# Attention, a dense layer and an expert layer on one core: every engine's part of an attention unit is given a slot of its own, and two other orders are changed with it

## The chip, the core and the metric

The kernel runs on one core of a Trainium2 chip. The core has five engines, each with an instruction queue of its own that is worked off in order: TensorE (PE), VectorE (DVE), ScalarE (ACT), GpSimd (POOL) and SyncE (SP), the last of which only issues transfers here. The metric is the device time of one execution in microseconds (us), lower is better. Engines wait for one another by semaphores alone, and the kernel writes each of these waits out by hand.

## What is computed

The reference, cut to what matters: a linear attention over 8 batches of 8 heads, a dense layer with `h - tanh(h)` in the middle, and a layer of 8 experts in which each token goes to one expert.

```python
q_s = softmax(q, axis=-1);  k_s = softmax(k, axis=2)        # q, k, v: (8, 8, 576, 64)
kv  = einsum('bhsd,bhde->...', k_s^T v);  a = q_s @ kv      # per head
x   = a.transpose(0, 2, 1, 3).reshape(4608, 512)
h   = x @ w_in;  x = (h - tanh(h)) @ w_out                  # 512 -> 2048 -> 512
logits = normed(x) @ normed(expert_emb).T / tau
e = argmax(logits);  gate = softmax(logits)[e]
out[n] = gate[n] * (relu(x[n] @ w1[e[n]]) @ w2[e[n]])       # 512 -> 1024 -> 512
```

All tensors are float32. Each matrix product of the two layers is done as three products of a high part and a low part (`split3`, lines 528 to 532: high times high, high times low, low times high), which keeps the accuracy of float32.

## The kernel before, in words

**Two halves.** The first half joins attention, dense layer and routing in one stream; the second is the expert layer.

**Slots.** The dense layer is cut into 12 blocks of 384 tokens and each block into 16 chunks of 128 of the 2048 inner columns: 192 chunks, one for each slot. In slot `s` PE does the first product of chunk `s+2` (12 matmuls of 384 columns), the second product of chunk `s` (9 matmuls of 512 columns), then what attention and routing have for it. ACT and DVE do the elementwise work of chunk `s+2`: on ACT a square, a tanh, a second square, the rounding of the chunk before to `g_hi`, and a mask (lines 799 to 811); on DVE four operations (lines 1000 to 1008). POOL makes `g_lo` of chunk `s+1` (L1397). The second product waits for `g_lo`; the first product of a chunk waits for the last DVE operation of the chunk two before. A turn of 48 slots (`SUPER`) covers three blocks, that is two batches. `walk` (line 370) writes out 16 slots, then a loop of three turns, then the last 32 slots.

**Attention units.** A unit is two heads of one batch; there are 32. Units 0 to 4, and the first steps of unit 5, are done in a prologue, whose order is the list `PROLOGUE`; the others lie beside the dense layer. `unit_at` (line 283) gives each of them four slots in a row: the eight units of a turn take slots 28 to 47 and 0 to 11, and slots 12 to 27 have none. Within the four slots `STAGES` (line 83) says what is done in which, the same for PE, DVE and POOL, with a shorter list for ACT. A `+` means the next unit:

- slot 0: `qa` (PE turns half of q, ACT copies it), `kT` (PE turns the folded k, DVE takes the maximum, L1032), `qmax` of the next unit (DVE maximum L1019, POOL subtracts it L1408)
- slot 1: `row` (PE spreads the maximum, DVE subtracts it L1035, ACT exponential L828), `qb` (the other half of q), `qexp` of the next unit (ACT L831)
- slot 2: `kv` (PE 12 pairs of small matmuls L602, DVE scales them L1039 to L1045), `qsum` of the next unit (DVE L1022 to L1026, POOL multiplies L1412)
- slot 3: `out` (PE two matmuls L608 and L609, ACT rounds both halves L834 and L836, DVE takes the rests L1049 and L1052), `kfold` of the next unit (DVE L1029)

All units share two accumulator banks, A and Bk. In the last turn the steps with `+` run once more, for a unit 32 that does not exist, on data that SP loads a second time for it.

**Routing.** The block that has just been finished is routed in the 16 slots of the next one. `ROUTE` gives each step its slot: three times `turn`, `pieces`, `logits`, with PE, ACT and DVE handing one bank to and fro (L620, L849, L1069, L852, L1072, L640), then `choose` on DVE in slot 9, `ranks` in slot 10, `dest` on DVE in slot 11 (L1107 to L1118), and one scatter of 128 rows on POOL in each of the slots 11, 12 and 13 (L1424). In slot 15 POOL waits until the scatters have landed and says so with `rows_free`; ACT waits for that before it writes the next block's rows into the same tile (`rows_out`, line 857).

**The order inside a slot** is the same on each engine: elementwise work, then attention, then routing. In the first 12 slots of all, ACT and DVE also split ten pieces of the weights (`SPLITS`, L869 and L1132).

**The expert layer** has 37 tiles of 128 rows that are live. PE does for tile `t`: first half of the hidden product of `t+1`, the transposes of `t` (L713), those of `t+2` (L685), second half of the hidden product of `t+1`, second product of `t`. DVE does for tile `t`: a test whether weights are to be split, `h_split` (L1219), `t_split` of `t+2` (L1213), more tests and splits of weights (L1337), then `scaled` (L1346), which waits for the second product and writes the output tile. In a loop of seven rounds four tiles are written out; the jump back to its top stands on DVE between `scaled` of one tile and `h_split` of the next.

Of the kernel before, what the change touches and what calls it, by code (L numbers as in the profile page):

```python
# [80 lines left out]
    "w:4 emb:0 first:0 kv:4 qmax:5 w:5 qa:4 first:1 qb:4 qexp:5 emb:1 qsum:5 out:4 kfold:5").split())]  # L81

STAGES = ("qa", "kT", "qmax+"), ("row", "qb", "qexp+"), ("kv", "qsum+"), ("out", "kfold+")
STAGES_ACT = (("qa",), ("qb", "row", "qexp+"), (), ("out",))
# [11 lines left out]
         11: ("dest", "scatter:0"), 12: ("scatter:1",), 13: ("scatter:2",), 15: ("stored",)}  # L96
# [23 lines left out]
def build(nc, q, k, v, w_in, w_out, emb, tau, w1, w2, ident_d, tri_d, cst_d, rows_d, pad_d, out):  # L120
# [91 lines left out]
    def unit_bufs(u, par):  # L212
# [42 lines left out]
    rows_free, route_step, oneh_ready, shift_ready, p_exp, rank_ready, dest_ready, rows_stored = (  # L255
        sem(x) for x in ("rows_free", "route_step", "oneh_ready", "shift_ready", "p_exp", "rank_ready", "dest_ready", "rows_stored"))
# [26 lines left out]
    def unit_at(m, s):  # L283

        if s >= 28:
            j = 2 * UPB + (s - 28) // 4
        elif s < 12:
            j = UPB + 1 + s // 4
        else:
            return None  # L290
        if isinstance(m, int) and 2 * UPB * m + j >= UNITS:
            return None
        return m * (2 * UPB) + j, s % 4, j // UPB % 2, j % UPB, j % 2
# [56 lines left out]
    def steps_of(stages, u, stage_, hf, c, par, part):  # L350

        for x in stages[stage_]:
            if x[-1] == "+":
                part(x[:-1], u + 1, hf, c, 1 - par)
            else:
                part(x, u, hf, c, par)

    def prologue(part, piece_, first, emb_):

        for x, i in PROLOGUE:  # L360
            if x == "w":
                piece_(i)
            elif x == "first":
                first(i)
            elif x == "emb":
                emb_(i)
            else:
                part(x, i, i // UPB, i % UPB, i % 2)
# [25 lines left out]
    def _(sp):  # L394
# [71 lines left out]
        sp.wait_ge(q_normed, UNITS + 1)  # L466
        sp.wait_ge(kfolded, UNITS + 1)
# [57 lines left out]
    def _(pe):  # L525
# [38 lines left out]
        def attention(m, s):  # L564
            at_ = unit_at(m, s)
            if at_:
                attention_stage(*at_)

        def attention_stage(u, stage_, hf, c, par):
            steps_of(STAGES, u, stage_, hf, c, par, part)  # L570

        def part(what, u, hf, c, par):

            q_, k_, v_, kv_, qT_, kfold_, _, _, kmax_, _, bankA, bankB = unit_bufs(u, par)
            if what == "qa":
                pe.wait_ge(q_normed, u + 1)
                if not isinstance(u, int) or u >= UPB:
                    pe.wait_ge(xlo_b, u + 1)
# [3 lines left out]
            elif what == "kT":  # L582
                pe.wait_ge(kfolded, u + 1)
                if not isinstance(u, int) or u >= UPB:
                    pe.wait_ge(xlo_a, u)
                nc.tensor.transpose(bankA[:, 0:SP], kfold_[:], ident[0:SP, 0:SP]).then_inc(kmaxT_ready, 1)
            elif what == "row":

                pe.wait_ge(kmax_done, u + 1)
                nc.tensor.transpose(bankA[0:SP, 0:P], kmax_[:, 0:1].broadcast_to([P, SP]),  # L590
# [76 lines left out]
        def slot(m, s):  # L667
# [3 lines left out]
            attention(m, s)  # L671
# [106 lines left out]
    def _(act):  # L778
# [34 lines left out]
        def attention_stage(u, stage_, hf, c, par):  # L813
            steps_of(STAGES_ACT, u, stage_, hf, c, par, part)

        def part(what, u, hf, c, par):
# [15 lines left out]
            elif what == "out":  # L832
                act.wait_ge(oa_ready, u + 1)
                nc.scalar.copy(x_hi[:, c, col:col + HALF], bankA[:, 0:HALF]).then_inc(xhi_a, 1)  # L834
                act.wait_ge(ob_ready, u + 1)
# [21 lines left out]
        def rows_out(m, s):  # L857
# [3 lines left out]
            act.wait_ge(rows_free, j + 1)  # L861
# [11 lines left out]
        def slot(m, s):  # L873
# [4 lines left out]
            at_ = unit_at(m, s)  # L878
            if at_:
                attention_stage(*at_)  # L880
# [101 lines left out]
    def _(dve):  # L982
# [27 lines left out]
        def attention_stage(u, stage_, hf, c, par):  # L1010
            steps_of(STAGES, u, stage_, hf, c, par, part)

        def part(what, u, hf, c, par):
# [16 lines left out]
            elif what == "kT":  # L1030
                dve.wait_ge(kmaxT_ready, u + 1)
                V.tensor_reduce(kmax_[:, 0:1], bankA[:, 0:SP], axis=AX.X, op=ALU.max).then_inc(kmax_done, 1)  # L1032
# [14 lines left out]
            elif what == "out":  # L1047
                dve.wait_ge(xhi_a, u + 1)
                V.tensor_tensor(x_lo[:, c, col:col + HALF], bankA[:, 0:HALF],  # L1049
                                x_hi[:, c, col:col + HALF].bitcast(F32), ALU.subtract).then_inc(xlo_a, 1)  # L1050
                dve.wait_ge(xhi_b, u + 1)
# [114 lines left out]
        def slot(m, s):  # L1166
# [4 lines left out]
            at_ = unit_at(m, s)  # L1171
            if at_:
                attention_stage(*at_)
# [175 lines left out]
        def slot(t, j, ahead1, ahead2, stored):  # L1349
            with live(dve, t):  # L1350
                if ahead1:

                    weights(t, T_SOLE, range(4))
                h_split(t, j)
                if ahead2:
                    with live(dve, t + 2):
                        t_split(t + 2, (j + 2) % 4)
# [136 lines left out]
```

## Time and profile before

| | us |
|---|---|
| median of 3 runs (1533.52 to 1538.3) | 1535.5 |
| the profiled execution | 1540.79 |
| its span, first to last instruction | 1539.0 |
| PE busy in the span | 1442.9 (94%) |
| DVE busy | 920.7 (60%) |
| ACT busy | 768.3 (50%) |
| POOL busy | 397.7 (26%) |
| mean granted clock of PE, as a share of full speed | 0.981 |

The slot work runs from 61 us to about 1025 us of the span, the expert layer from there to the end. A busy time is the sum of the durations of an engine's instructions where they do not overlap. Matmuls overlap, since one starts before the one ahead has ended, so short waits of PE don't show in its busy time; they show in the distance between starts.

### The profile page before, as it was taken

What the parts mean: (1) busy time and instruction counts of PE and PEld (TensorE: products, weight loads), DVE (VectorE), ACT (ScalarE), POOL (GpSimd) and SP (SyncE); (2) the same over time, 40 slices, a digit from 0 to 9 for tenths busy, and PEclk for the clock granted to TensorE, in tenths of its full rate; (3) what the DMA queues carried; (4) which work ended last, traced back from release to release, by engine and by line L of the source; (5) the groups of instructions that cost most, each with busy time, mean ns of one, the idle gap of its engine ahead of it and who ended that gap; (6) DMA issues with size and microseconds to landing.
All of it is one profiled execution on the core that took longest, in us unless ns stands there. A gap on an engine that the chain in (4) does not pass through costs nothing.

```text
span 1539.0 us, 27343 instructions
## 1 busy us (share of the span) xinstructions
PE 1442.9 (94%) x8080; PEld 1226.6 (80%) x8081; DVE 920.7 (60%) x1784; ACT 768.3 (50%) x1559; POOL 397.7 (26%) x348
## 2 busy tenths in 40 slices
PE   4799999999999999999999999999999899899996
PEld 3678888888888888888888888877888778678785
DVE  7886677878577878667887766675314123232221
ACT  3666666675657666656666566652323123132220
POOL 3433233334233343324333323231000000000000
PEclk9899999999999999999999999998999999999999
DMA  9532012212001221101121002025312211311110
GB/s 193 148 94 79 1 45 47 64 36 53 9 25 44 47 68 34 37 1 52 42 65 40 22 1 76 1 97 193 116 44 90 94 42 53 131 34 47 41 39 25
DMA packets 139524, 91.18 MB, mean 59 GB/s; under 512 B 118873, under 2 KB 119129, under 8 KB 139233
## 3 DMA queue, kind: packets, MB, share of 16 engines
q1 hardware_dynamic: 132784, 70.12, 17.1%
q0 software_dynamic: 5840, 18.92, 3.3%
q8 instruction: 64, 1.05, 0.3%
q14 instruction: 100, 0.81, 0.2%
q10 hardware_dynamic: 736, 0.29, 0.1%
HBM read 70.39 MB, written 21.28 MB: 60 GB/s over the span
## 4 chain that ended last, share of the span: by engine, by line
PE 56%; DVE 22%; issue 10%; ACT 6%; POOL 3%; DMA 1%; DVEq 1%; ACTq 1%; SPq 0%; POOLq 0%
PE ps L530 17%; PE ps L531 17%; PE ps L532 17%; DVE gs L1003 5%; DVE gs L1000 2%; DVE kfold L1029 2%; ACT gs L804 2%; DVE gs L1008 2%; PE ps L713 2%; DVE k_sb L1035 2%; DVE qrec L1022 1%; POOL g_lo L1397 1%; DVE ps L1001 1%; ACT q_sb L831 1%; PE ps L685 1%
## 5 line engine op out<-in xcount | busy, mean ns | idle before, releaser
L1397 POOL TENSOR_TENSOR g_lo<-gs,g_hi 128x384 fp32r<-128x384 f32 x192 | 205.3, 1069 | 420.2 <-ACT g_hi L809 419.0
L530 PE MATMUL ps<-x_hi,wi_hi 128*128 128x384 f32 x768 | 277.0, 361 | 0.8 <-issue 0.8
L531 PE MATMUL ps<-x_lo,wi_hi 128*128 128x384 f32 x768 | 261.4, 340 | 0.0
L532 PE MATMUL ps<-x_hi,wi_lo 128*128 128x384 f32 x768 | 261.2, 340 | 0.0
L530 PE MATMUL ps<-wo_hi,g_hi 128*128 128x512 f32 x576 | 233.1, 405 | 26.5 <-POOL g_lo L1397 26.2
L531 PE MATMUL ps<-wo_lo,g_hi 128*128 128x512 f32 x576 | 231.0, 401 | 0.0
L532 PE MATMUL ps<-wo_hi,g_lo 128*128 128x512 f32 x576 | 229.6, 399 | 0.0
L799 ACT ACTIVATE usq<-ps 128x384 f32<-128x384 f32 x192 | 93.8, 488 | 250.8 <-PE ps L532 250.8
L920 ACT ACTIVATE hb<-ps 128x512 f32<-128x512 f32 x74 | 44.3, 598 | 330.9 <-PE ps L532 330.9
L1000 DVE SCALAR_TENSOR_TENSOR gs<-gs,ps 128x384 f32<-128x384 f32 x192 | 106.0, 552 | 169.0 <-ACT gs L804 167.5
L1003 DVE TENSOR_TENSOR gs<-gs,usq 128x384 f32<-128x384 f32 x192 | 175.4, 914 | 0.0
L530 PEld LDWEIGHTS ps<-wo_hi,g_hi 128*128 128x128 f32 x576 | 109.5, 190 | 54.9 <-POOL g_lo L1397 24.1
L1466 POOL DMA_INDIRECT out<-osb,xrow x37 | 36.2, 979 | 448.1 <-DVE osb L1346 431.0
L530 PEld LDWEIGHTS ps<-x_hi,wi_hi 128*128 128x128 f32 x768 | 145.8, 190 | 5.9 <-issue 1.7
L531 PEld LDWEIGHTS ps<-x_lo,wi_hi 128*128 128x128 f32 x768 | 145.9, 190 | 2.9
L532 PEld LDWEIGHTS ps<-x_hi,wi_lo 128*128 128x128 f32 x768 | 145.4, 189 | 0.0
L1346 DVE TENSOR_SCALAR osb<-ps,xrow 128x512 f32<-128x512 f32 x37 | 27.8, 750 | 188.5 <-PE ps L532 188.5
L530 PE MATMUL ps<-w_hi,h_hi 128*128 (+1 forms) x296 | 120.6, 408 | 18.3 <-DVE h_lo L1219 18.3
L1008 DVE COPY_PREDICATED gs<-big,ps 128x384 f32<-128x384 uint16 x192 | 114.3, 595 | 34.0 <-DVE gs L1003 34.0
L532 PEld LDWEIGHTS ps<-wo_hi,g_lo 128*128 128x128 f32 x576 | 109.6, 190 | 26.8
L530 PE MATMUL ps<-w_hi,t_hi 128*128 (+1 forms) x296 | 122.0, 412 | 2.6 <-issue 2.6
L531 PEld LDWEIGHTS ps<-wo_lo,g_hi 128*128 128x128 f32 x576 | 109.3, 190 | 17.5
(209 smaller groups left out, 2698.8 us busy)
## 6 DMA issues: line engine op xcount, KB each, us to landing
w_raw<-w SPq DMA_DIRECT2D x10, 2048.0 KB, 9.0
xrow<-scratch SPq DMA_DIRECT2D x37, 257.0 KB, 2.7
q_sb<-q SPq DMA_DIRECT2D x62, 144.0 KB, 3.0
k_sb<-k SPq DMA_DIRECT2D x62, 144.0 KB, 3.1
v_sb<-v SPq DMA_DIRECT2D x60, 144.0 KB, 3.3
in_raw<-w_in SPq DMA_DIRECT2D x8, 512.0 KB, 5.9
out_raw<-w_out SPq DMA_DIRECT2D x8, 512.0 KB, 5.6
scratch<-pad_d SPq DMA_DIRECT2D x8, 257.0 KB, 4.5
```

Source lines behind the costliest of these rows:

```text
L530: mm(out_, a_hi, b_hi, start=first, stop=False)
L531: mm(out_, a_hi, b_lo, start=False, stop=False)
L532: return mm(out_, a_lo, b_hi, start=False, stop=last)
L713: last = nc.tensor.transpose(ps[:, 3 + b, i * P:(i + 1) * P], hb[:, j % 2, (4 * b + i) * P:(4 * b + i + 1) * P], ident[:])
L799: fn(usq[:, s % 2], h, ACT.Square).then_inc(u_ready, 1)
L804: fn(gs[:, s % 2], usq[:, s % 2], ACT.Square, bias=cst[:, C_BIAS:C_BIAS + 1], scale=SQ_SCALE).then_inc(s_ready, 1)
L920: fn(hb[:, j % 2, 512 * hf:512 * (hf + 1)], ps[:, 1 + hf], ACT.Relu).then_inc(relu_done, 1)
L1000: V.scalar_tensor_tensor(g, g, SQ_REST, h, ALU.add, ALU.mult).then_inc(poly_step, 1)
L1003: V.tensor_tensor(g, g, u, ALU.mult).then_inc(poly_ready, 1)
L1008: V.copy_predicated(g, big[:].bitcast(U16), h).then_inc(g_ready, 1)
L1397: G.tensor_tensor(g_lo[:, (s - 1) % 3], gs[:, (s - 1) % 2], g_hi[:, (s - 1) % 3].bitcast(F32), ALU.subtract).then_inc(glo_ready, 1)
L1466: G.indirect_dma_start(out, bass.IndirectOffsetOnAxis(ap=xrow[:, j, DEST:DEST + 1].bitcast(U32), axis=0), osb[:, j], None, bounds_check=N ...
```

## The change

Attention no longer goes by stages of four slots. A table `EVENTS` names for each engine its operations and, for each, a distance in slots from the unit's last slot, called `t`. A unit now spreads over eight slots, from `t-6` to `t+1`. `out` is cut in two: `outa` at `t`, `outb` at `t+1`. The operations of one engine follow in the order of its row; an operation of POOL or ACT lies one slot or more behind that of DVE or PE whose result it takes, and the other way round, in most cases.

| operation | slots before, from `t` | slots after |
|---|---|---|
| `qmax` | -7 | DVE -6, POOL -5 |
| `kfold` | -4 | DVE -5 |
| `qexp` | -6 | ACT -4 |
| `kT` | -3 | PE, DVE -4 |
| `qsum` | -5 | DVE -4, POOL -3 |
| `row` | -2 | PE, DVE -3, ACT -2 |
| `qa` | -3 | PE, ACT -2 |
| `qb` | -2 | PE, ACT -1 |
| `kv` | -1 | PE, DVE -1 |
| `out` | 0 | first half 0, second half +1 |

`kT` now uses bank Bk, and the waits on the banks follow from that: `row` waits until `outa` of the unit before is read, `outb` until the maximum of the unit behind it is taken. The prologue ends with `kT:5`. The steps for unit 32 and their loads are gone, and SP loads the first expert's weights when the last unit has been read. In routing `dest` moves from slot 11 to 12, the scatters from 11, 12, 13 to 13, 13, 14; POOL's wait in slot 15 is gone, and ACT waits for the scatters itself. In the expert layer DVE's loop begins elsewhere: its body is `scaled` of a tile and then the splits of the next, so that the jump back stands between the splits of a tile and its `scaled`. The order of DVE's work is the same.

The diff, cut to its core:

```diff
-    "w:4 emb:0 first:0 kv:4 qmax:5 w:5 qa:4 first:1 qb:4 qexp:5 emb:1 qsum:5 out:4 kfold:5").split())]
-STAGES = ("qa", "kT", "qmax+"), ("row", "qb", "qexp+"), ("kv", "qsum+"), ("out", "kfold+")
-STAGES_ACT = (("qa",), ("qb", "row", "qexp+"), (), ("out",))
+    "w:4 emb:0 first:0 kv:4 qmax:5 w:5 qa:4 first:1 qb:4 qexp:5 emb:1 qsum:5 out:4 kfold:5 kT:5").split())]
+EVENTS = dict(
+    PE=(("kT", -4), ("row", -3), ("qa", -2), ("qb", -1), ("kv", -1), ("outa", 0), ("outb", 1)),
+    ACT=(("qexp", -4), ("row", -2), ("qa", -2), ("qb", -1), ("outa", 0), ("outb", 1)),
+    DVE=(("kT", -4), ("qsum", -4), ("row", -3), ("qmax", -6), ("kv", -1), ("kfold", -5), ("outa", 0), ("outb", 1)),
+    POOL=(("qmax", -5), ("qsum", -3)))
...
-         11: ("dest", "scatter:0"), 12: ("scatter:1",), 13: ("scatter:2",), 15: ("stored",)}
+         12: ("dest",), 13: ("scatter:0", "scatter:1"), 14: ("scatter:2",)}
...
-    def unit_at(m, s):
+    def attention(engine, m, s, part):
+        for what, after in EVENTS[engine]:
+            turn, t = divmod(s - after, SUPER)
+            if t % 4 != 3 or 12 <= t < 28:
+                continue
+            j = 2 * UPB + (t - 28) // 4 if t >= 28 else UPB + 1 + t // 4
+            if isinstance(m, int) and not UPB < (m + turn) * 2 * UPB + j < UNITS:
+                continue
+            part(what, (m + turn) * (2 * UPB) + j, j // UPB % 2, j % UPB, j % 2, t)
...
-        sp.wait_ge(qTb_ready, UNITS - 1)
-        load(q_sb[:, 0], q_d, q_in, 0, 0)
-        sp.wait_ge(kv_ready, UNITS - 1)
-        load(k_sb[:, 0], k_d, k_in, 0, 0)
...
-        sp.wait_ge(q_normed, UNITS + 1)
-        sp.wait_ge(kfolded, UNITS + 1)
+        sp.wait_ge(qTb_ready, UNITS)
+        sp.wait_ge(kv_ready, UNITS)
         sp.wait_ge(first_known, 1)
...
             if what == "qa":
                 pe.wait_ge(q_normed, u + 1)
+                pe.wait_ge(kmax_done, u + 1)
...
             elif what == "kT":
                 pe.wait_ge(kfolded, u + 1)
+                if t in (None, 31):
+                    if u >= UPB if isinstance(u, int) else True:
+                        pe.wait_ge(xlo_b, u + 1)
+                else:
+                    pe.wait_ge(qTb_copied, u)
+                nc.tensor.transpose(bankB[:, 0:SP], kfold_[:], ident[0:SP, 0:SP]).then_inc(kmaxT_ready, 1)
+            elif what == "row":
+                pe.wait_ge(kmax_done, u + 1)
                 if not isinstance(u, int) or u >= UPB:
                     pe.wait_ge(xlo_a, u)
-                nc.tensor.transpose(bankA[:, 0:SP], kfold_[:], ident[0:SP, 0:SP]).then_inc(kmaxT_ready, 1)
...
-            elif what == "out":
+            if what in ("outa", "out"):
                 pe.wait_ge(kvb_ready, u + 1)
+                pe.wait_ge(qTa_copied, u + 1)
+                mm(bankA[:, 0:HALF], kv_, qT_[:, 0:HALF], start=True, stop=True).then_inc(oa_ready, 1)
+            if what in ("outb", "out"):
                 pe.wait_ge(qTb_copied, u + 1)
-                mm(bankA[:, 0:HALF], kv_, qT_[:, 0:HALF], start=True, stop=True).then_inc(oa_ready, 1)
+                if t not in (None, 11):
+                    pe.wait_ge(kmax_done, u + 2)
                 mm(bankB[:, 0:HALF], kv_, qT_[:, HALF:S], start=True, stop=True).then_inc(ob_ready, 1)
...
-            act.wait_ge(rows_free, j + 1)
+            if not isinstance(j, int) or j > 0:
+                act.wait_ge(rows_stored, j * (16 * GPB))
...
-        slot(3, 3, True, True, None)
+        splits(3, 3, True, True)
+        scaled(3, 3, None)
+        splits(4, 0, True, True)
         with dve.Fori(1, LOOPS) as i:
             for j in range(4):
-                slot(i * 4 + j, j, True, True, i * 16)
+                scaled(i * 4 + j, j, i * 16)
+                splits(i * 4 + (j + 1), (j + 1) % 4, True, True)
+        scaled(4 * LOOPS, 0, 16 * LOOPS)
```

`splits` is the old DVE `slot` of the expert layer without its last line, the call of `scaled`. ACT, DVE and POOL split their `part` for `out` in the same way as PE.

## Rows read from the trace of the kernel before

**Rows 1.** Waits of PE over the whole span: us in total, times, longest.

```profile
PE ps L530 <- POOL g_lo L1397: 26.2, 26, 2.4
PE ps L530 <- DVE h_lo L1219: 18.3, 7, 5.8
```

**Rows 2.** Stretches: from:to, length, busy us of PE, PEld, DVE, ACT, POOL, clock, DMA.

```profile
61.24:137.69 76.45, 68.20 (x383) 57.57 (x383) 63.17 (x106) 47.16 (x92) 33.37 (x20) 0.96 0.34 91
203.88:396.91 193.03, 184.36 (x1160) 159.06 (x1160) 151.57 (x314) 122.11 (x263) 73.36 (x63) 0.99 0.20 50
296.06:315.80 19.74, 19.74 (x121) 17.44 (x121) 15.13 (x30) 14.50 (x32) 9.38 (x8) 1.00 0.28 75
450.42:641.80 191.38, 182.64 (x1160) 157.97 (x1160) 151.54 (x314) 122.00 (x263) 73.16 (x63) 1.00 0.20 51
695.20:887.52 192.32, 183.97 (x1160) 159.19 (x1159) 151.63 (x314) 122.04 (x263) 73.19 (x63) 0.99 0.17 44
887.52:958.25 70.73, 70.67 (x394) 62.89 (x394) 46.67 (x102) 43.36 (x96) 20.52 (x20) 1.00 0.11 38
949.82:958.25 8.43, 8.43 (x43) 7.61 (x43) 5.70 (x15) 6.04 (x13) 2.02 (x2) 1.00 0.72 251
```

**Rows 3.** Timeline of DVE, a third slot of a unit and the fourth behind it.

```profile
263.27 0.14 DVE L1039 TENSOR_SCALAR krec<-ps 128x1 f32<-128x1 f32 x1
...
264.26 0.95 DVE L1022 TENSOR_REDUCE qrec<-q_sb 96x12 f32<-96x768 f32 x1
...
265.81 0.55 DVE L1000 SCALAR_TENSOR_TENSOR gs<-gs,ps 128x384 f32<-128x384 f32 x1
...
268.30 0.44 DVE L1049 TENSOR_TENSOR x_lo<-ps,x_hi 128x288 fp32r<-128x288 f32 x1
...
269.02 1.54 DVE L1029 TENSOR_REDUCE kfold<-k_sb 96x128 f32<-96x768 f32 x1
```

**Rows 4.** Timeline of DVE, first operation on a chunk in the slot from 949.82.

```profile
951.42 0.55 DVE L1000 SCALAR_TENSOR_TENSOR gs<-gs,ps 128x384 f32<-128x384 f32 x1 [0.73 <-ACT gs L804]
```

**Rows 5.** Timeline of ACT, DVE and PE, first hand-overs of a block's routing.

```profile
235.29 0.84 ACT L828 ACTIVATE k_sb<-k_sb 96x768 f32<-96x768 f32 x1 [2.23 <-DVE k_sb L1035]
...
237.37 0.70 DVE L1069 TENSOR_TENSOR ps<-ps,y 128x512 f32<-128x512 f32 x1 [2.11 <-ACT y L849]
...
244.37 0.29 PE L640 MATMUL ps<-en,y 128*128 128x24 bf16 x5 [0.84 <-DVE y L1072]
```

**Rows 6.** Timeline of POOL and PE, scatter of a block and the slot behind it.

```profile
379.70 1.06 POOL L1424 DMA_INDIRECT scratch<-yrow,dest  x1 [4.39 <-DVE dest L1118]
...
381.85 0.74 PE L530 MATMUL ps<-wo_hi,g_hi 128*128 128x512 f32 x1 [2.01 <-POOL g_lo L1397]
```

**Rows 7.** Timeline of PE and DVE, end of the prologue and first slot.

```profile
57.11 0.94 PE L530 MATMUL ps<-x_hi,wi_hi 128*128 128x384 f32 x1
...
62.22 1.55 DVE L1029 TENSOR_REDUCE kfold<-k_sb 96x128 f32<-96x768 f32 x1
63.70 1.21 DVE L1132 TENSOR_TENSOR wi_lo<-in_raw,wi_hi 128x1024 fp32r<-128x1024 f32 x1
```

**Rows 8.** The line of the 36 scatters (L1424), its transfers.

```profile
DMA to landing us min/median/max: 3.3/3.9/8.0
```

**Rows 9.** Stretches of the expert layer: 22 tiles with the jumps, 3 without.

```profile
1141.09:1439.54 298.45, 282.90 (x1321) 230.55 (x1320) 84.47 (x100) 80.63 (x122) 21.54 (x22) 0.97 0.21 67
1452.04:1489.55 37.51, 37.51 (x182) 30.85 (x180) 7.92 (x12) 7.96 (x15) 2.94 (x3) 1.00 0.13 41
```

**Rows 10.** Chain that ended last, at a jump: start, us, what (DVEq: DVE's sequencer).

```profile
1198.19 3.12 issue
...
1202.12 5.44 issue
```

**Rows 11.** Timeline of DVE, a tile without a jump ahead of it.

```profile
1096.38 0.75 DVE L1346 TENSOR_SCALAR osb<-ps,xrow 128x512 f32<-128x512 f32 x1 [6.71 <-PE ps L532]
1100.28 1.29 DVE L1219 TENSOR_TENSOR h_lo<-ps,h_hi 128x512 fp32r<-128x512 f32 x2 [3.15 <-ACT h_hi L925]
```

More of the change, by code:

```diff
@@ L367, in prologue @@
             else:
-                part(x, i, i // UPB, i % UPB, i % 2)
+                part(x, i, i // UPB, i % UPB, i % 2, None)
     def walk(eng, slot, extra={}):
@@ L562, in second_product, with part @@
             last.then_inc(l2_done, 1)
[L564 to L572, printed above, removed]
+        def part(what, u, hf, c, par, t):
             q_, k_, v_, kv_, qT_, kfold_, _, _, kmax_, _, bankA, bankB = unit_bufs(u, par)
@@ L670, in slot @@
             second_product(m, s)
-            attention(m, s)
+            attention("PE", m, s, part)
             if isinstance(m, int) and m == 0 and s == AHEAD - 1:
@@ L831, in part @@
                 fn(q_, q_, ACT.Exp).then_inc(q_exp, 1)
-            elif what == "out":
+            if what in ("outa", "out"):
                 act.wait_ge(oa_ready, u + 1)
                 nc.scalar.copy(x_hi[:, c, col:col + HALF], bankA[:, 0:HALF]).then_inc(xhi_a, 1)
+            if what in ("outb", "out"):
                 act.wait_ge(ob_ready, u + 1)
@@ L877, in slot @@
             elementwise(m + (s + 2) // SUPER, (s + 2) % SUPER)
-            at_ = unit_at(m, s)
-            if at_:
-                attention_stage(*at_)
+            attention("ACT", m, s, part)
             at_ = route_at(m, s)
@@ L1046, in part @@
                 last.then_inc(kvb_ready, 1)
-            elif what == "out":
+            if what in ("outa", "out"):
                 dve.wait_ge(xhi_a, u + 1)
@@ L1050, in part @@
                                 x_hi[:, c, col:col + HALF].bitcast(F32), ALU.subtract).then_inc(xlo_a, 1)
+            if what in ("outb", "out"):
                 dve.wait_ge(xhi_b, u + 1)
@@ L1170, in slot @@
             elementwise(m + (s + 2) // SUPER, (s + 2) % SUPER)
-            at_ = unit_at(m, s)
-            if at_:
-                attention_stage(*at_)
+            attention("DVE", m, s, part)
             at_ = route_at(m, s)
@@ L1347, in scaled, with splits @@
                             ALU.mult).then_inc(o_ready, 1)
[L1349 to L1357, printed above, removed]
-                if ahead1:
-                    weights(t, T_NEW, (0, 1))
-                    weights(t, T_SECOND, (2, 3))
-                scaled(t, j, stored)
+        def splits(t, j, ahead1, ahead2):
+            if ahead1:
+                weights(t, T_SOLE, range(4))
+            h_split(t, j)
+            if ahead2:
+                with live(dve, t + 2):
+                    t_split(t + 2, (j + 2) % 4)
+            if ahead1:
+                weights(t, T_NEW, (0, 1))
+                weights(t, T_SECOND, (2, 3))
         dve.wait_ge(tab_ready, 1)
@@ L1375, in _ @@
         scaled(2, 2, None)
-        slot(3, 3, True, True, None)
+        splits(3, 3, True, True)
+        scaled(3, 3, None)
+        splits(4, 0, True, True)
         with dve.Fori(1, LOOPS) as i:
             for j in range(4):
-                slot(i * 4 + j, j, True, True, i * 16)
-        for t in range(4 * LOOPS, TILES):
-            slot(t, t % 4, t + 1 < TILES, t + 2 < TILES, 16 * (t // 4))
+                scaled(i * 4 + j, j, i * 16)
+                splits(i * 4 + (j + 1), (j + 1) % 4, True, True)
+        scaled(4 * LOOPS, 0, 16 * LOOPS)
+        for t in range(4 * LOOPS + 1, TILES):
+            with live(dve, t):
+                splits(t, t % 4, t + 1 < TILES, t + 2 < TILES)
+                scaled(t, t % 4, 16 * (t // 4))
     @block.gpsimd
@@ L1409, in part @@
                                 ALU.subtract).then_inc(q_centred, 1)
-            elif what == "qsum":
+            elif what == "qsum" and not (isinstance(u, int) and u == UPB + 1 and t is not None):
                 pool.wait_ge(qrec_ready, u + 1)
@@ L1443, in slot @@
             lo(mm_, s2)
-            at_ = unit_at(m, s)
-            if at_:
-                attention_stage(*at_)
+            attention("POOL", m, s, part)
             at_ = route_at(m, s)
```

39 lines of the change are left out of this document (6 added, 33 removed).

## The prediction, made before the changed kernel was run

> **What bounds the kernel now.** I read the stretches first, then PE's waits, then the timeline at the places where these end. PE is the bound: where a stretch has neither attention nor routing, two slots take 8.43 us, 4.22 each, and PE is busy for all of it [rows 2]. So time can be won only where PE stands still, and I measure that by lengths. Sixteen slots with routing and no attention take 70.73, so routing adds 70.73 - 16 x 4.22 = 3.2. Four slots of attention without routing and without a wait take 19.74, so a unit adds 19.74 - 4 x 4.22 = 2.86 [rows 2]. The three spans of 36 slots around the attention of a turn hold 8 units and 2 routings each: 36 x 4.22 + 8 x 2.86 + 2 x 3.2 = 181.2. They take 193.0, 191.4 and 192.3 [rows 2], which leaves 11.8 + 10.2 + 11.1 = **33.1 us** of standing still. The first 13 slots hold 3 units and no routing: 54.9 + 8.6 = 63.5 against 76.45, so **13.0**. In the expert layer three tiles take 37.51, 12.50 each; the 22 tiles from 1141.09 on take 298.45 where 22 x 12.50 = 275.0 [rows 9]: **23.4**. PE's waits have two large entries, for POOL's `g_lo` and for DVE's `h_lo` [rows 1]; the first belongs to the slots, the second to the expert layer.
>
> DVE comes close behind. It is busy for 151.6 of 193.0 us in a span, 79% [rows 2]. As starts go, an elementwise chunk takes 268.30 - 265.81 = 2.49 of it, `kv` 0.99, `qsum` 1.55 with 0.1 of that a routing step, `out` 0.72 [rows 3], `kfold` 63.70 - 62.22 = 1.48 [rows 7]; `row` and `qmax` are one pass over 96 x 768 elements like L1022, 0.9 each.
>
> **Where the spans stand still.** First hand-over: ACT waits 2.23 for DVE's `row` of the same slot, then does both exponentials, 0.84 each, and only then routing's copy, so DVE waits 2.11 for that copy, and PE 0.84 for `logits` seven microseconds on [rows 5]. Second: `dest` ends late because `out`, `kfold` and `dest` meet in slot 11 on DVE; POOL waits 4.39 with its scatter at the head of the queue, `g_lo` stands behind it, and PE waits 2.01 for that [rows 6].
>
> **The change, spans.** Per four slots DVE's attention work was, in order, 1.1, 0.9, 2.4, 2.2. Now it is 1.3 (`row`, `outb`), 0.9 (`qmax`), 2.5 (`kv`, `kfold`), 2.0 (`kT`, `qsum`, `outa`): the same sum, as even as before. What is better is what it meets. `dest` (some ten small operations, 0.14 and a gap each like L1039 [rows 3], so 1.5 to 2, an estimate) falls on a slot with 1.3 instead of 2.2, and the scatters one slot later find it done, so POOL no longer stands with `g_lo` behind it. ACT's exponential of k finds its input a slot old, the other exponential is in another slot, and routing's copy no longer queues behind a wait. POOL's `qsum` no longer waits in the slot in which DVE makes it. I then went through each wait of PE with a slot of 4.9 to 5.5 and DVE's first operation 1.6 after PE's slot begins (951.42 against 949.82 [rows 2, 4]): `kT`, `qa`, `qb`, `kv`, `outa` and `outb` each find their inputs 1 us old or more. The closest is `row`, which needs `outa` of the unit before out of the bank: DVE is through with it 1.6 + 2.5 + 2.0 = 6.1 after the slot begins, PE comes for it at 4.9 + 2.1 = 7.0. DVE's worst slot is the one with `choose` (2.5 + 0.9 + some 2.3 for ten linked small operations, 5.7 against 4.9 for PE), and the next ones give that back. So I keep 1.5 of stall per span and take 33.1 - 4.5 = **28.6 us**. Bounds: 33.1, and half, 16.
>
> **The change, start.** Here it costs something first. The prologue now ends with `kT:5`, and on PE this stands ahead of the first product of chunk 2, which started at 57.11; it needs `kfold:5`, which DVE runs from 62.22 to 63.8 [rows 7]. PE stands for 6.8 us, and resumes at 1.2 instead of 2.4 GHz, as it had it here anyway: from 57.11 to the next product at 61.24 its 12 matmuls took 4.1 us, where 4.22 is otherwise enough for 21 [rows 2, 7]. The second product of chunk 0 moves from 61.24 to about 68. But DVE uses these microseconds for two pieces of the weights that were in the way later, and POOL's two waits no longer stand before `g_lo`. Taking slot by slot the later of PE (4.22 and its attention) and of DVE (2.5, attention, 1.2 for each weight piece [rows 7]), I get 82.6 for the start of slot 3, 103.4 for slot 7, 128.3 for slot 12 and 133.1 for slot 13, which was at 137.69: **4.6 us** won of 13.0. Bounds: -4 (the delay is kept) and 9.
>
> **Scatters and the end of the slots.** Each scatter takes 3.9 us to land, up to 8.0 [rows 8]. The third one is now issued in slot 14, after POOL's `qmax` where there is one, and ACT waits for its landing itself in slot 15 before `rows_out`; behind ACT's wait stands the next chunk's square, and behind the copies PE's second product of the next slot. With 3.9 it lands about 1 us after ACT asks, with PE still 1 us short of needing the copies: no cost inside the turns. At the last block nothing follows that could absorb it, the weights of the first expert load at the same time, and the scatter behaves like the 8.0 one: I charge **-2 us** (bounds 0 and -5). The removed work for unit 32 lay beside a full PE and saves nothing; SP's first weight load still waits for `first_known`, which was the later condition.
>
> **Expert layer.** At six places DVE jumps back between `scaled` and `h_split`. In an ordinary tile `h_split` starts 3.90 after `scaled` and the 3.15 before it are spent waiting for ACT [rows 11]. At a jump two gaps of issue come in between, 3.12 and 5.44 at the longest [rows 10], and PE waits, 18.3 in seven waits [rows 1], the seventh being the last tile, which stays. Moved behind the splits, the jump falls into the 6.71 us that DVE waits for the second product anyway [rows 11]; the output tile has a tile's time to spare. All of 23.4 goes, and I take **22.5**, with 16 as the lower bound: the second gap stands at the test for weights (the jump over a skipped block), and that test still follows `scaled`.
>
> That second gap is where a page speaks against the change. The Trainium skill, "Runtime: NRT & Kernel Launch", section Instruction fetch mechanics, says that prefetch is sequential and that a taken branch to a target outside the current window of two pages forces a fetch before execution goes on. By it the skip over the weight block costs its fetch wherever it stands, and only the first gap is hidden. The trace agrees that both jumps have a gap; whether the second needs the first ahead of it, it does not show.
>
> Sum: 28.6 + 4.6 - 2 + 22.5 = 53.7. The profiled execution took 1540.8, so 1487.1; the median lies 5.3 below that execution, so **1482**.
>
> **Rivals.** (a) *DVE holds the spans.* Its in-order waits come back at other places, `choose` and the pairs of `kv` and `kfold` push its elementwise work late, and half of the 33.1 stays. For it: 79% busy, and its share rises to 84% when the span shrinks. Against: only the slot with `choose` holds clearly more work for DVE than for PE. 28.6 becomes 16: 1494. (b) *The second gap stays in the expert layer.* At the jump of rows 10 the second gap ends at 1207.56; 3.12 earlier is 1204.4, 6.2 behind the begin of the first gap, where an ordinary `h_split` stands 3.9 behind `scaled`, so it is still 2.4 late [rows 10, 11]; a gap of 3.12 or less fits into the 3.15. Over the six jumps I keep a quarter of 23.4, 6 us: 1488. The Trainium skill's page named above, "Runtime: NRT & Kernel Launch", gives this case. (c) *The shared bank.* `row` of a unit waits on PE until DVE has read `outa` of the one before, which it does last of three operations. Slack is 0.9. If DVE runs 2.9 us late there, PE stands 2.0 per unit, and a product at half clock behind it costs some 2 more (the 4.1 above against half of it): 27 units x 4 = 108 us, 1482 + 108 = 1590. It passes the old time from a loss of 53.5 / 27 = 2.0 us per unit on. Against: DVE's lateness adds up to 0.8 in my count. (d) *Nothing to speak of*: what the spans win is lost at the start and at the end, and the fetch keeps its place: 1535.
>
> **How the numbers follow.** My forecast 0.60, (a) 0.18, (b) 0.13, (c) 0.05, (d) 0.04. The low end takes all upper bounds, 33.1 + 9 + 23.4 = 65.5, so 1470, and 2 for the spread of runs: 1468. The high end is (a) and (b) together, 1500, with 3 for the last block: 1503. A measurement of this kernel tells 0.3% from no change, about 5 us. Faster: forecast, (a), (b) and a little of (d), 0.92; same 0.03; slower 0.05.
>
> **What would show it.** PE's waits without L1219 except once; the 22 tiles 275 to 277 long. Three spans of 36 slots (now with their events from slot 25 on) 182 to 184 long, no wait for `g_lo` behind a scatter. One wait of 6 to 7 us at `kT` (L586 before) near 57 us, and slot 13 at about 133. ACT waiting for the scatter at the last block. Wrong would be: waits of PE at `row`, a DVE without gaps through the spans, issue gaps still ahead of `h_lo`.

## The result, and the profile after

The changed kernel takes **1485.7 us** (median of four runs, 1484.5 to 1490.0) against 1534.5 for the one before in the same session (four runs, 1533.0 to 1538.3): ratio 0.9683, with a 95% interval of 0.9656 to 0.9710. The forecast was 1482, with a range of 1468 to 1503. The profiled execution took 1489.95 us, 50.8 less than the one of before (1540.8), and the terms below are differences between these two.

I read the same stretches as before, each set between two events that both kernels have. The three spans of attention are taken from slot 25 to slot 64 of their turn here, since the new events begin earlier than the old stages. First, stretches of the kernel before, the three spans and the last 15 slots ahead of the last one (from:to, length, busy us of PE, PEld, DVE, ACT, POOL, clock, DMA):

```profile
190.48:396.91 206.43, 197.76 (x1244) 170.85 (x1244) 161.28 (x338) 129.09 (x279) 76.38 (x66) 0.99 0.19 47
437.02:641.75 204.73, 195.99 (x1244) 169.71 (x1244) 161.26 (x338) 128.98 (x279) 76.20 (x66) 1.00 0.19 47
681.86:887.52 205.66, 197.31 (x1243) 170.93 (x1243) 161.29 (x338) 129.03 (x279) 76.22 (x66) 0.99 0.16 41
958.25:1023.45 65.20, 63.27 (x353) 54.99 (x352) 42.72 (x86) 39.88 (x86) 21.04 (x19) 1.00 0.11 31
```

Then stretches of the changed kernel: the first 13 slots, the three spans, the 16 slots with routing alone, the 15 slots behind them, the 22 expert tiles:

```profile
66.50:130.09 63.59, 63.59 (x381) 56.40 (x381) 53.47 (x93) 45.21 (x90) 20.85 (x17) 0.99 0.38 106
182.88:378.69 195.81, 193.43 (x1244) 170.86 (x1243) 163.30 (x338) 126.99 (x279) 78.61 (x66) 1.00 0.20 50
418.78:614.05 195.27, 193.49 (x1243) 170.84 (x1243) 162.03 (x338) 126.68 (x279) 78.32 (x66) 1.00 0.20 50
654.16:849.96 195.80, 193.49 (x1244) 170.91 (x1243) 162.09 (x338) 126.55 (x279) 78.39 (x66) 1.00 0.16 40
849.96:924.35 74.39, 70.57 (x395) 62.82 (x394) 47.09 (x102) 42.60 (x95) 20.62 (x20) 1.00 0.12 40
924.35:992.22 67.87, 64.42 (x353) 56.37 (x353) 44.20 (x87) 42.82 (x89) 20.26 (x18) 0.97 0.09 25
1110.37:1385.41 275.04, 275.04 (x1322) 226.36 (x1320) 84.21 (x100) 80.65 (x122) 21.52 (x22) 1.00 0.22 72
```

The spans lost 10.6, 9.5 and 9.9 us, 29.9 together; PE now stands still in them for 2.4, 1.8 and 2.3 (length less busy), where it was 8.7, 8.7 and 8.4; the rest of the gain is in PE's busy time itself, 193.5 for 197.0 on average, since a short wait doesn't show as one. The expert tiles take 275.04 for 298.45 [rows 9], and PE is busy for every microsecond of them: 23.4 won. Slot 13 begins at 130.09 instead of 137.69 [rows 2]: 7.6 won. One stretch went the other way: the 16 slots with routing alone take 74.39 instead of 70.73 [rows 2]; the 15 slots behind them take 67.87 where it was 65.2, so the end of the slots costs 6.3 in all. From the second product of the last expert tile to the end of the span it is 18.5 us instead of 15.3, 3.1 more. Added up: 7.6 + 29.9 - 6.3 + 23.4 - 3.1 = 51.5, within 0.7 of the 50.8.

Two of these terms compare one execution with one, and other runs vary there. The prologue before slot 0 is the same in `before` as in three runs shown below (before_pad, rot_only, route_only), and slot 0 begins at 61.24 in the one and at 58.80, 58.95 and 58.99 in the others. PE's lines of before and before_pad:

```profile
61.24 0.40 PE L530 MATMUL ps<-wo_hi,g_hi 128*128 128x512 f32 x1
58.80 0.40 PE L530 MATMUL ps<-wo_hi,g_hi 128*128 128x512 f32 x1
```

So some 2.3 of the 7.6 us belong to the profiled execution of before and not to the change, which leaves about 5.3 for the change. And the stretch from the last second product to the end is 15.0 to 15.3 us in eight of the profiled runs and 17.0 to 18.5 in the six others. Of the ten with the new events four are in the first group (no_rot 15.2) and six in the second (events_only 18.1); the four with the old ones are all in the first, so whether the change has a part in it stays open. PE waits 2.7 us for `h_lo` ahead of it before and after the change; the six microseconds from its begin have a granted clock of 0.72 after and of 1.00 before:

```profile
1469.44:1475.44 6.00, 6.00 (x19) 4.78 (x20) 0.00 (x0) 0.00 (x0) 0.00 (x0) 0.72 0.08 29
1523.69:1529.69 6.00, 5.86 (x24) 4.42 (x24) 0.11 (x1) 0.00 (x0) 0.00 (x0) 1.00 0.07 24
```

Waits of PE in the changed kernel (us in total, times, longest), which answer to [rows 1]:

```profile
PE ps L571 <- DVE kfold L1014: 25.3, 9, 9.0
PE ps L519 <- ACT yrow L853: 5.4, 4, 3.8
PE ps L640 <- DVE oneh L1089: 4.2, 4, 1.5
PE ps L519 <- POOL g_lo L1384: 3.5, 2, 2.6
PE ps L519 <- DVE h_lo L1203: 2.7, 1, 2.7
```

POOL's `g_lo` fell from 26 waits to two, both in the last block, and `h_lo` from seven to the one of the last tile. New is a wait for `yrow`, ACT's copies of the next block's rows: 3.8 us at the end of the slots, and 1.6 us in three short waits inside the turns. The first entry is the prologue, and in it the wait at `kT:5` that was forecast as 6.8 us. Timeline of PE at that place:

```profile
62.38 0.42 PE L571 MATMUL ps<-ident,kfold 96*128 96x96 f32 x1 [6.97 <-DVE kfold L1014]
```

Where the end of the slots loses time, the timeline of ACT and PE (slot 176 of 191), then of POOL, DVE and ACT in the last block:

```profile
923.62 1.56 ACT L853 COPY yrow<-ps 128x512 f32<-128x512 f32 x3 [4.99 <-DMA scratch<-yrow,dest]
924.35 0.72 PE L519 MATMUL ps<-wo_hi,g_hi 128*128 128x512 f32 x1 [3.82 <-ACT yrow L853]
...
988.00 2.29 DVE L1165 TENSOR_TENSOR w_lo<-w_raw,w_hi 128x2048 fp32r<-128x2048 f32 x1
988.37 2.76 POOL L1408 DMA_INDIRECT scratch<-yrow,dest  x1 [0.30 <-issue]
992.04 2.29 DVE L1165 TENSOR_TENSOR w_lo<-w_raw,w_hi 128x2048 fp32r<-128x2048 f32 x1 [1.11 <-ACT w_hi L878]
992.22 0.50 PE L519 MATMUL ps<-wo_hi,g_hi 128*128 128x512 f32 x1 [2.62 <-POOL g_lo L1384]
992.33 2.87 POOL L1408 DMA_INDIRECT scratch<-yrow,dest  x1 [0.17 <-issue]
999.32 1.56 ACT L853 COPY yrow<-ps 128x512 f32<-128x512 f32 x3 [7.30 <-DMA scratch<-yrow,dest]
```

And the timeline of SP and POOL 9 us ahead of the first of these waits:

```profile
914.19 0.41 SPq L450 DMA_DIRECT2D w_raw<-w  x1
915.14 1.12 POOL L1408 DMA_INDIRECT scratch<-yrow,dest  x1 [0.16 <-issue]
```

The third scatter of the block is issued 0.95 us after the first 2 MB load of expert weights and is through at 923.6, some 8.5 us later, where the median was 3.9 [rows 8]. ACT waits 4.99 for it, PE 3.82 for ACT, and PE then works at a granted clock of 0.72 for the next 5 us, so partly at 1.2 instead of 2.4 GHz:

```profile
925.00:930.00 5.00, 5.00 (x20) 4.29 (x19) 2.47 (x4) 4.42 (x12) 1.01 (x1) 0.72 0.01 3
```

In the last block two scatters take POOL 2.8 us each, beside DVE's split of weights, where the usual one took 1.06 [rows 6]; each ends some 0.85 us behind DVE's operation.

### The profile page after: what moved, and what is told of

Same layout as the page of the kernel before. It is cut to its first block, busy times and chain, and to the rows that moved or that the text cites. A ratio compares the mean times of both kernels' runs of the same rounds, so it can differ in the third digit from the quotient of the medians.

```text
span 1487.9 us, 27350 instructions
## 1 busy us (share of the span) xinstructions
PE 1421.7 (96%) x8080; PEld 1223.4 (82%) x8081; DVE 920.1 (62%) x1779; ACT 759.4 (51%) x1558; POOL 395.3 (27%) x346
## 3 DMA queue, kind: packets, MB, share of 16 engines
q1 hardware_dynamic: 130416, 69.53, 17.9%
## 4 chain that ended last, share of the span: by engine, by line
PE 79%; DVE 7%; issue 6%; POOL 3%; DMA 3%; ACT 1%; SPq 0%; DVEq 0%; POOLq 0%; ACTq 0%
PE ps L519 24%; PE ps L520 23%; PE ps L521 23%; PE ps L704 2%; DMA scratch<-yrow,dest 2%; PE ps L589 1%; POOL g_lo L1384 1%; PE ps L676 1%; PE ps L611 1%; PE ps L600 1%; DVE gs L991 1%; PE ps L595 1%; DMA xrow<-scratch 1%; DVE kfold L1014 1%; POOL q_sb L1392 1%
## 5 line engine op out<-in xcount | busy, mean ns | idle before, releaser
L1384 POOL TENSOR_TENSOR g_lo<-gs,g_hi 128x384 fp32r<-128x384 f32 x192 | 194.6, 1014 | 590.4 <-ACT g_hi L800 590.3
L519 PE MATMUL ps<-x_hi,wi_hi 128*128 128x384 f32 x768 | 280.1, 365 | 1.1 <-issue 1.1
L519 PE MATMUL ps<-wo_hi,g_hi 128*128 128x512 f32 x576 | 229.7, 399 | 8.9 <-ACT yrow L853 5.4
```

Source lines behind the costliest of these rows:

```text
L519: mm(out_, a_hi, b_hi, start=first, stop=False)
L1384: G.tensor_tensor(g_lo[:, (s - 1) % 3], gs[:, (s - 1) % 2], g_hi[:, (s - 1) % 3].bitcast(F32), ALU.subtract).then_inc(glo_ready, 1)
```

## The experiments

The experiments ran in three sessions, in which the kernel before gave medians of 1535.1, 1536.3 and 1534.3 us; each ratio is against the one it ran with. Differences of some 5 us between two experiments are near what the intervals of the ratios can tell; where one is used below, the trace is asked too.

### The parts one by one

**rot_only**: the kernel before with the new beginning of DVE's expert loop.

```diff
-                slot(i * 4 + j, j, True, True, i * 16)
+                scaled(i * 4 + j, j, i * 16)
+                splits(i * 4 + (j + 1), (j + 1) % 4, True, True)
```

> The kernel before with DVE's expert loop begun elsewhere and nothing else. Theory (the jump's gaps are hidden behind the wait for the second product): the 22 tiles from the second product of tile 7 to that of tile 29 take 275 to 276 us instead of 298.5, the slots are untouched, the time falls by 22 to 24 us to about 1512. Rival (b) (the gap at the test for weights stays behind scaled): 281 us or more for the 22 tiles, time 1518 or more, and issue gaps ahead of h_lo.

1514.3 us, ratio 0.9865 (0.9830 to 0.9899). The tiles all take 12.50, the slots are as before. That fits a jump whose gaps are hidden; it fits gaps that are gone just as well, and the next part shows that they were gone.

**route_only**: the kernel before with `dest` and the scatters later and ACT waiting for them itself.

```diff
-         11: ("dest", "scatter:0"), 12: ("scatter:1",), 13: ("scatter:2",), 15: ("stored",)}
+         12: ("dest",), 13: ("scatter:0", "scatter:1"), 14: ("scatter:2",)}
...
-            act.wait_ge(rows_free, j + 1)
+            if not isinstance(j, int) or j > 0:
+                act.wait_ge(rows_stored, j * (16 * GPB))
```

> The kernel before with dest and the scatters one slot later and ACT waiting for the scatters itself; attention in its old stages, expert loop as before. Theory (two causes in the spans: dest and the scatter at the head of POOL's queue, and hand-overs inside a slot): the waits for g_lo in slots 44, 60 and 61 of a turn go, some 4 to 5 us for each turn, the waits at logits stay (6.4 us in the span); at the last two blocks 5 to 7 us are lost to late scatters. Time 1534.5 - 13 + 6 = 1527, between 1522 and 1533. Rival: the events alone bring the gain and this part is worth nothing: 1538 or more.

1568.1 us, ratio 1.0214 (1.0187 to 1.0241): slower by 33 us, and not faster by 8. The timeline of POOL, ACT and PE, two slots of the first turn, shows why:

```profile
221.15 1.47 POOL L1412 TENSOR_TENSOR q_sb<-q_sb,qrec 96x768 f32<-96x768 f32 x1 [3.57 <-DVE qrec L1027]
222.78 1.14 POOL L1424 DMA_INDIRECT scratch<-yrow,dest  x1 [0.16 <-issue]
226.27 1.56 ACT L864 COPY yrow<-ps 128x512 f32<-128x512 f32 x3 [4.86 <-DMA scratch<-yrow,dest]
226.91 0.50 PE L530 MATMUL ps<-wo_hi,g_hi 128*128 128x512 f32 x1 [3.81 <-ACT yrow L864]
```

With the old stages POOL's `qsum` waits 3.57 for DVE in the very slot in which the third scatter now is, and the scatter goes out behind it, at 222.78. The new slots of the scatters are right only with the new events, in which POOL's `qsum` has its input already.

**route_old**: the changed kernel with `dest` and the scatters in their old slots 11, 12 and 13.

```diff
-         12: ("dest",), 13: ("scatter:0", "scatter:1"), 14: ("scatter:2",)}
+         11: ("dest", "scatter:0"), 12: ("scatter:1",), 13: ("scatter:2",)}
```

> The changed kernel with dest in slot 11 and the scatters in 11, 12, 13 again, ACT still waiting for them itself. Theory: in the spans POOL waits for dest again with g_lo behind it, but dest now meets 2.0 of attention work on DVE instead of 2.2, so 3 to 5 us are lost per turn, 9 to 14 in all; at the last two blocks 6 us are won back. Time 1485.7 + 12 - 6 = 1491, between 1486 and 1497. Rival (the later slots only cost, since the events have made room on DVE): 1482 or less.

1484.0 us, ratio 0.9657 (0.9628 to 0.9686), no slower than the changed kernel, and below the 1491 that was expected. The two halves cancel: in each turn two slots at a scatter take 5.8 and 5.7 where they took 4.3 and 4.8, at the end the 16 slots are back at 70.7.

**end_early** keeps the new slots in the turns and takes the old ones for the last two blocks.

```diff
-        for x in ROUTE.get(stage_, ()):
+        for x in (ROUTE_END if isinstance(j, int) and j >= NBLK - 3 else ROUTE).get(stage_, ()):
```

`ROUTE_END` is `ROUTE` with the old slots of these steps.

> The changed kernel, but dest and the scatters of the last two blocks of four units at their old slots (dest and first scatter in slot 11, then 12 and 13); all blocks in the turns keep the new slots. Theory LATE END (the second half of the change costs nothing in the turns and about 6 us behind them, where the scatters land behind the 2 MB load of w1 or beside DVE's weights): the wait of 3.8 us in slot 175 and those of the last block shrink, 1479 to 1481. Rival (the waits only move to another engine): 1484 to 1487.

1478.3 us, ratio 0.9622 (0.9593 to 0.9651): 7.5 below the changed kernel. Its stretches of the last 31 slots, ACT's waits for the scatters, and the same waits in the changed kernel:

```profile
848.00:918.70 70.70, 70.64 (x394) 62.90 (x394) 46.65 (x102) 43.32 (x96) 20.51 (x20) 1.00 0.11 39
918.70:983.90 65.20, 63.28 (x353) 55.04 (x352) 43.51 (x87) 40.71 (x87) 21.05 (x19) 1.00 0.11 30
```

```profile
ACT yrow L854 <- DMA scratch<-yrow,dest: 7.6, 9, 3.4
```

```profile
ACT yrow L853 <- DMA scratch<-yrow,dest: 18.9, 10, 7.3
```

So the later scatters gain 1484.0 - 1478.3 = 5.7 us in the turns and lose 7.5 behind them. The traces agree on the size: slots 0 to 159 take 789.8 us in route_old, 783.5 in the changed kernel and 781.6 in end_early, and the 31 slots behind them 135.9 in route_old and end_early against 142.3 in the changed kernel.

**events_only**: the changed kernel with both other parts undone, so the attention events alone (the edits of route_old, and the reverse of that of rot_only).

> The changed kernel with only the attention events new: DVE's expert loop and the slots of dest and the scatters are as before the change. The loop starts at 1632 of DVE's stream. If the events alone bring the three spans, the start and (by place) the expert layer: 1481 to 1485, tiles all 12.5 us, q14 near 68 packets. If the parts need one another (the earlier single undoings each covered for the other): 1490 to 1510.

1485.5 us, ratio 0.9682 (0.9666 to 0.9698), the whole gain of the change.

### The expert loop: where the wait went

**no_rot**: the changed kernel with DVE's expert loop as it was before.

> The changed kernel with DVE's expert loop as before. Theory: the parts are independent, the 22 tiles take 298 us again, the time is 1485.7 + 23.5 = 1509, within 3. If it were less than 1503 or more than 1515, the loop's gain would hang on what the slots do.

1484.6 us, ratio 0.9673 (0.9646 to 0.9700), not 1509. The tiles took 12.50 each although the jump stood in its old place. So the gaps had gone without any hiding, and the forecast's "hidden behind the 6.71 us" was not needed to explain the changed kernel.

The packets of queue q14, over which instructions are loaded, divided the kernels: 100 before and 98 in route_only, both with gaps, 68 or 69 in all without. I counted DVE's compiled instructions up to the top of the loop, which has 312 (313 when rotated): 1643 before and in route_only, 1632 in no_rot, 1695 after, 1706 in rot_only. The new events give DVE 11 instructions less, the rotation puts the top 63 later. So the runs are divided by the loop's place as well: gaps at 1643, none at 1632, 1695 and 1706.

The Trainium skill, "Runtime: NRT & Kernel Launch", section Instruction fetch mechanics, says that the instruction memory holds two blocks of 256 instructions and that a jump out of them forces a fetch. By it a loop of 312 that lies over three blocks can never stay in and one over two can. With the 256 of the Trainium skill's page the counts then bound the border B between two blocks, as an estimate: the loop from 1632 ends at 1943 and must end ahead of B + 256, so B is above 1687, and the loop at 1695 must not begin ahead of it, so B is at most 1695. Three kernels tested the place: the kernel before, no_rot and the changed kernel, each with a block ahead of the loop whose condition is false, so that only the loop's place is moved, to 1704, 1653 and 1912:

```diff
+        with dve.If(entry(0, T_SECOND, 1) > 0):
+            for _ in range(55):
+                hold(dve)
```

(55 for before_pad, 15 for no_rot_pad, 211 for after_pad; the test adds six instructions in each.) By the estimate the loop lies over two blocks at 1704 and over three at 1653 and at 1912, which is 1656 + 256.

> The kernel before, with a block of DVE instructions behind the third product of the expert layer that is never executed (its condition is false), so that nothing is changed but where the DVE's expert loop lies in its instruction stream: 61 instructions later (start at 1704 instead of 1643). Theory PLACE (the gap at the jump is a fetch of instructions that is made anew each round only where the loop's 312 instructions of 64 bytes touch three pages of 256, which the loop at 1643 does and the loops at 1632, 1695 and 1706 do not): the gaps go, expert tiles all 12.5 us, about 1513 us, and the instruction queue q14 falls from 100 packets to about 68. Theory WORK (the gap hangs on what DVE or ACT had done before, so on the work and not on the place): as before, 1535, 100 packets.

1514.3 us, ratio 0.9864 (0.9833 to 0.9894). Moved by 61 instructions that never run, the kernel before wins 22 us, as much as by the rotation.

> The changed kernel with DVE's expert loop as before the change (the run of 1484.6 us whose tiles had no gaps), and a never executed block of 21 instructions ahead of the loop, so that it starts at 1653, between the place with gaps (1643) and those without (1695). Theory PLACE: the gaps come back, as in the kernel before, one tile in four 3 to 8 us longer, about 1508 us, q14 at about 100 packets. Theory WORK: 1485, 68 packets.

1502.5 us, ratio 0.9779 (0.9750 to 0.9809). The gaps are back, at a smaller sum than before: 17.9 us over no_rot. Its chain of waits at a jump, which answers to [rows 10] (issue is time in which DVE waits for nothing that the trace shows):

```profile
1165.48 3.17 issue
...
1169.47 5.62 issue
...
1175.20 0.07 DVE h_lo L1203
```

> The changed kernel with a never executed block of 217 instructions ahead of DVE's expert loop, which then starts at 1912 = 1656 + 256, so touches three pages by theory PLACE and is fetched anew each round. It tells what the rotation of the loop is worth where the fetch is there. If the first gap is hidden behind DVE's wait for ACT and no second gap follows (my forecast's mechanism): about 1486, q14 at about 100. If the second gap stays (rival (b) of the prediction): one tile in four 1 us longer or more, 1490 to 1495. If nothing is hidden: about 1508. By theory WORK: 1486 and 68 packets.

1486.7 us, ratio 0.9674 (0.9643 to 0.9704). The fetches are there and cost next to nothing. q14 in the stretch from 1090 to 1440 (packets, MB, share), first of before, then after_pad, then after; before_pad has 5 there:

```profile
q14 instruction: 34, 0.28, 0.3%
```

```profile
q14 instruction: 34, 0.28, 0.3%
```

```profile
q14 instruction: 4, 0.03, 0.0%
```

At one jump, behind a split of weights, DVE of after_pad came late to it, and a gap of 1.48 before `h_lo` held PE for 1.45 us; the 22 tiles take 276.76 there for 275.04. Timeline of DVE:

```profile
1326.65 4.49 DVE L1321 TENSOR_TENSOR w_lo<-w_raw,w_hi 128x2048 f32 x2 [6.08 <-ACT w_hi L904]
1331.73 0.75 DVE L1330 TENSOR_SCALAR osb<-ps,xrow 128x512 f32<-128x512 f32 x1 [0.58 <-issue]
1333.96 1.29 DVE L1203 TENSOR_TENSOR h_lo<-ps,h_hi 128x512 fp32r<-128x512 f32 x2 [1.48 <-issue]
```

With the fetches present the rotation is worth 1502.5 - 1486.7 = 15.8 us; with them absent nothing (no_rot 1484.6, after 1485.7). The three new places came out as the estimate said. That the border is where I put it in the chip's memory is still inferred, from seven places of the loop, four without and three with gaps or fetches; nothing here reads it. The Trainium skill's page and the runs agree that a jump can force a fetch, and that the same jump need not.

### The spans and the start

**exp_same_slot**: ACT's exponential of k one slot earlier, in the slot in which DVE makes its input.

```diff
-    ACT=(("qexp", -4), ("row", -2), ("qa", -2), ("qb", -1), ("outa", 0), ("outb", 1)),
+    ACT=(("qexp", -4), ("row", -3), ("qa", -2), ("qb", -1), ("outa", 0), ("outb", 1)),
```

> The changed kernel with one of ACT's events moved: the exponential of k (row on ACT) at -3, in the slot in which PE spreads the maximum and DVE subtracts it, and not one slot later. Theory SLOT BETWEEN (the spans gain because a result is taken a slot after it is made): ACT stands before its exponential and is late for the next g_hi, each span grows by 2 to 10 us, 1492 to 1510. Rival (the spans gain from fewer slots that hold too much work, whatever the distance; ACT at about half busy takes the wait): 1485 to 1488.

1520.2 us, ratio 0.9911 (0.9894 to 0.9927): one entry of the 23 in `EVENTS`, moved one slot, takes back 34.5 us, more than the 24 I allowed. ACT's waits over the whole span, the timeline of ACT and PE at one unit, and the stretch behind a wait for `choose`:

```profile
ACT k_sb L816 <- DVE k_sb L1020: 82.4, 29, 7.3
```

```profile
472.64 0.85 ACT L816 ACTIVATE k_sb<-k_sb 96x768 f32<-96x768 f32 x1 [2.62 <-DVE k_sb L1020]
476.02 0.65 PE L611 MATMUL ps<-ident,yrow 128*128 128x128 f32 x4 [1.18 <-ACT ps L833]
526.20 0.18 PE L640 MATMUL ps<-oneh,tri 128*128 128x8 bf16 x1 [1.94 <-DVE oneh L1089]
```

```profile
527.00:532.00 5.00, 5.00 (x19) 4.54 (x18) 4.14 (x10) 2.16 (x5) 0.30 (x1) 0.66 0.49 108
```

ACT stands 2.62 with routing's squares (L833) behind it, PE gets them 1.18 late; in the slot of `choose` DVE's `oneh` is 1.94 late, and the five microseconds behind that have a granted clock of 0.66. The 16 slots from slot 32 of a turn grow from 81.5 to 88.5, the 16 behind them from some 79.4 to 82.1.

**kT_in_slot**: the `kT` of unit 5 is taken on PE in slot 0 and not at the end of the prologue.

```diff
+            if isinstance(m, int) and (m, s) == (0, 0):
+                part("kT", UPB + 1, 1, 1, (UPB + 1) % 2, None)
```

> The changed kernel, but PE's part of kT of unit 5 is taken out of the end of the prologue, where PE waits 7.0 us for DVE's kfold, and done in slot 0 after the second product. If that wait is what delays slot 0: 4 to 6 us less, 1480 to 1482. Rival (slot 0 and 1 then wait for DVE in its place): 1484 to 1487.

1481.6 us, ratio 0.9653 (0.9636 to 0.9671), 4.2 less. The interval overlaps that of the changed kernel, but the trace has slot 13 at 126.9 instead of 130.1. Slot 0 begins at 58.5, not 66.5, but the slots behind it take 68.4 and not 63.6: the rest of DVE's lateness is met there. Timeline of PE:

```profile
61.54 0.30 PE L571 MATMUL ps<-ident,kfold 96*128 96x96 f32 x1 [0.61 <-DVE kfold L1020]
```

**best** joins end_early and kT_in_slot.

> end_early (1478.3) and kT_in_slot together: if the two add, 7.5 us below the changed kernel and what kT_in_slot gains, so 1473 to 1478; if kT_in_slot gains nothing, as end_early.

1473.6 us (1473.4 to 1475.2), ratio 0.9610 (0.9594 to 0.9626): 12 us below the changed kernel; the two add up. It is the fastest version found.

## Why the prediction came out right

**Spans, 28.6 forecast, 29.9 measured.** The mechanism held: a result is taken a slot after it is made. exp_same_slot shows it by its reverse for one of the events; the others were not moved singly. By events_only the events need neither of the other parts. Of the 33.1 us of standing still, 33.1 - 29.9 = 3.2 are left, 1.1 per span where I had kept 1.5. The largest wait in them is the one at `choose`, which I had named as DVE's one bad slot: it holds PE at `oneh` for 0.9 in each. Rival (a), DVE as the bound, fell: DVE is busy for 83%, as it said, and PE stands for only 2.2 per span all the same. Rival (c) fell too: PE has no wait at `row` in the spans.

**Start, 4.6 forecast, 7.6 measured.** The wait at `kT:5` was 6.97 for 6.8 forecast. The product behind it began at 66.50, not 68, and the 13 slots took 63.59, PE busy throughout, where my slot by slot count had 65.1. The second half of the term was 1.5 too careful. The first was not: I had read `kfold:5` at 62.22 from an execution whose prologue ran 2.3 us late, and the changed kernel's prologue did not. Against the other executions of the old prologue slot 0 came 7.5 us later (66.5 for 59.0), where I had forecast 6.8, and the whole term is 5.3 for 4.6.

**Scatters and end, -2 forecast, -6.3 measured.** The step "no cost inside the turns" held but for the 1.6 us at `yrow`: on the whole the later slots win 5.7 us there. What failed is the size at the end. I had priced the last block alone. The block before it pays too, since its third scatter comes behind the first 2 MB load of weights, 3.8 us of PE and a slot partly at half clock; and in the last block POOL's scatters take 2.8 us beside DVE's `w_lo`, which I had not counted at all.

**Expert layer, 22.5 forecast, 23.4 measured.** The size was right, and in this it was lucky: the reason given was true but not the one that was needed. The rotation does hide the fetch, as after_pad shows. Of rival (b) the 1.45 us at the one late jump are left; at the other jumps `h_lo` starts 3.8 behind `scaled` as in any tile, so that a gap there is no longer than the some 3.1 us of waiting for ACT, where it was up to 5.44 before. Yet in the changed kernel there is nothing to hide. By their instruction count alone the new events move the loop to where it is not fetched anew, and the rotation moves it to another such place. A change that left the loop alone would have won the same 23.4 us, as no_rot and events_only show. The forecast had no term for the loop's place.

The last tile's 3.1 us were in no term; some runs with the new events have them and some don't. The errors were +1.3, +3.0, -4.3, +0.9 and -3.1, a sum of -2.2: the total came closer than its terms, and that is luck. Without what varies from execution to execution, the 2.3 at the start and the 3.1 at the end, the errors are +1.3, +0.7, -4.3 and +0.9, and the one that stands out is the end of the slots.

## What to carry to other kernels

A stall at a loop's jump may be a matter of where the loop lies in the instruction stream: look at the packets of the instruction queue, and pad with a block that never runs before explaining it by the work. Undoing one part of a change proves nothing where two parts each suffice; undo them together and alone. Before a difference of 2 or 3 us between two profiled executions is explained, look at the same stretch in a third kernel that shares it. A slot that is right for a step in the steady state can be wrong for the last blocks, where other queues load for the next stage: give the tail its own table.

## What was not expected of the hardware

- A loop of 312 or 313 instructions on DVE came with 34 packets of some 8 KB on the instruction queue in the stretch of the tiles at three places in the stream (1643, 1653, 1912), and with 4 to 6 at four others (1632, 1695, 1704, 1706). That is read as a fetch at every round. Where nothing covered it, there were gaps of issue at the jumps, up to 3.2 and 5.6 us.
- A scatter of 128 rows issued 0.95 us behind a 2 MB load took some 8.5 us to land, against a median of 3.9 [rows 8]; in end_early, where the scatters go out ahead of the load, ACT's longest wait for one is 3.4 instead of 7.3.
- Two indirect transfers took POOL 2.76 and 2.87 us to issue while DVE ran a two-input operation on 128 x 2048 elements, where 1.0 to 1.2 was usual; they ended 0.84 and 0.87 us behind that operation. The same two take 2.8 to 2.9 in all seven profiled kernels with the late scatters at the end, and none takes over 1.5 in the seven without, where none starts while that operation runs. That DVE's operation is the cause was not tested alone.
